# An mLSTM block ahead of two mixture-of-experts layers: decay products spread by DMA, a third bank for scores, output gates scaled on Pool, a new order of steps

## The reference, cut to what matters

```python
# attention part: batch 4, 8 heads, 768 tokens, head size 40
for t in range(S):
    m_new  = maximum(f_gate[t] + m, i_gate[t])
    f_stab = exp(f_gate[t] + m - m_new);  i_stab = exp(i_gate[t] - m_new);  m = m_new
    C = f_stab * C + i_stab * outer(v[t], k[t])
    n = f_stab * n + i_stab * k[t]
    y[t] = sigmoid(o_gate[t]) * (C @ q[t]) / maximum(abs(n @ q[t]), 1)
# then x = y as [3072, 320]; a capacity-limited top-1 MoE of 8 experts (320 -> 1024 -> 320, relu),
# then a second MoE routed by cosine similarity with a softmax weight.
```

## Time and profile before

| | us |
|---|---|
| median of the runs (972.93, 976.13, 2472.59) | 976.13 |
| profiled execution, its own time | 968.82 |
| its span | 967.0 |
| PE busy | 812.1 (84%) |
| DVE busy | 525.9 (54%) |
| POOL busy | 406.4 (42%) |
| ACT busy | 277.1 (29%) |
| mean granted clock of PE | 0.851 |

### The profile page before, as it was taken

One profiled execution on the slowest core, in us unless ns is written; L12 is line 12 of the kernel. 1 busy time (PEld: TensorE's weight loads), 2 busy tenths in 40 slices (PEclk: granted clock), 3 DMA queues, 4 the chain that ended last, 5 costly groups with the idle time before them and its releaser, 6 DMA issues.

```text
span 967.0 us, 19426 instructions
## 1 busy us (share of the span) xinstructions
PE 812.1 (84%) x5835; PEld 733.5 (76%) x5836; DVE 525.9 (54%) x1467; ACT 277.1 (29%) x671; POOL 406.4 (42%) x558
## 2 busy tenths in 40 slices
PE   1899888889567777778999999991899999999995
PEld 0777777777466667767999999991788888888994
DVE  7776878834776666666356666657222222222221
ACT  4221212200000000000467667663233332333331
POOL 4443434406510000001468888765043766527541
PEclk9998999969555555555999999996899999999999
DMA  5343444356931110115145555443547777762320
GB/s 151 122 131 116 137 128 144 113 161 168 366 98 65 65 64 34 65 65 177 49 145 165 164 164 164 140 141 104 153 136 209 219 192 249 215 194 77 104 94 1
DMA packets 72325, 131.78 MB, mean 136 GB/s; under 512 B 14583, under 2 KB 55936, under 8 KB 70498
## 3 DMA queue, kind: packets, MB, share of 16 engines
q1 hardware_dynamic: 53186, 88.72, 29.3%
q0 software_dynamic: 9600, 35.85, 11.9%
q10 hardware_dynamic: 9504, 6.79, 2.8%
HBM read 94.18 MB, written 15.24 MB: 113 GB/s over the span
## 4 chain that ended last, share of the span: by engine, by line
PE 55%; DVE 14%; issue 5%; ACT 2%; POOL 2%; DMA 0%; DVEq 0%; ACTq 0%; POOLq 0%; SPq 0%
PE bank L1442 8%; PE bank L1444 8%; PE bank L1443 8%; PE bank L1406 5%; PE bank L1419 4%; PE bank L1369 3%; PE bank L1469 3%; PE bank L1470 2%; PE bank L1471 2%; PE bank L1560 2%; DVE routing_arena L1009 1%; PE bank L1542 1%; PE bank L1541 1%; PE bank L1361 1%; PE bank L1474 1%
## 5 line engine op out<-in xcount | busy, mean ns | idle before, releaser
L1442 PE MATMUL bank<-w_hi,hT_hi 128*128 (+1 forms) x440 | 140.7, 320 | 6.4 <-DVE hT_lo L1103 3.4
L1443 PE MATMUL bank<-w_lo,hT_hi 128*128 (+1 forms) x440 | 136.7, 311 | 0.0
L1444 PE MATMUL bank<-w_hi,hT_lo 128*128 (+1 forms) x440 | 136.5, 310 | 0.0
L741 POOL TENSOR_TENSOR w_lo<-w_raw,w_hi 128x320 fp32r<-128x320 f32 x128 | 108.3, 875 | 16.9 <-ACT w_hi L489 16.0
L683 POOL DMA_INDIRECT routing_arena<-x_rows,routing_arena x24 | 23.3, 969 | 203.0 <-DVE routing_arena L1091 181.9
L710 POOL TENSOR_TENSOR w_lo<-w_raw,w_hi 128x256 fp32r<-128x256 f32 x128 | 95.5, 776 | 28.6 <-DMA w_hi<-w_raw 25.4
L1442 PEld LDWEIGHTS bank<-w_hi,hT_hi 128*128 128x128 f32 x440 | 82.8, 188 | 9.0 <-issue 9.0
L1443 PEld LDWEIGHTS bank<-w_lo,hT_hi 128*128 128x128 f32 x440 | 82.8, 188 | 0.0
L1444 PEld LDWEIGHTS bank<-w_hi,hT_lo 128*128 128x128 f32 x440 | 82.7, 188 | 0.0
L1178 DVE TENSOR_TENSOR xT_lo<-bank,xT_hi 128x256 fp32r<-128x256 f32 x31 | 13.2, 425 | 112.9 <-ACT xT_hi L561 112.9
L1103 DVE SCALAR_TENSOR_TENSOR hT_lo<-bank,hT_hi 128x384 fp32r<-128x384 f32 x64 | 35.7, 558 | 68.6 <-ACT hT_hi L504 65.7
(11 more groups left out here) (268 smaller groups left out, 1969.8 us busy)
## 6 DMA issues: line engine op xcount, KB each, us to landing
w_raw<-in_moe_w SPq DMA_DIRECT2D x16, 1280.0 KB
w_raw<-in_moe_w SPq DMA_DIRECT2D x16, 1024.0 KB
w_hi<-w_raw POOLq DMA_DIRECT2D x8, 1280.0 KB, 7.4
w_raw<-in_moe_w SPq DMA_DIRECT2D x32, 256.0 KB
w_hi<-w_raw POOLq DMA_DIRECT2D x8, 1024.0 KB, 6.8
mlstm_arena<-in_q SPq DMA_DIRECT2D x64, 120.0 KB
tokens<-in_moe_w2t SPq DMA_DIRECT2D x8, 768.0 KB, 4.2
turn_arena<-in_moe_w2t SPq DMA_DIRECT2D x8, 768.0 KB, 4.3
```

The source lines that it names most:

```text
L741: last = nc.gpsimd.tensor_tensor(w2_part(w2_lo, n)[:, k, :], w2_raw[:, k, :], w2_part(w2_hi, n)[:, k, :], ALU.subtract)
L1442: T.matmul(dst, a_hi, b_hi, start=first, stop=False)
L1443: T.matmul(dst, a_hi, b_lo, start=False, stop=False)
L1444: return T.matmul(dst, a_lo, b_hi, start=False, stop=last)
```

## The change

- `cum_parts`, `sel_pair`, `ends` and `spread_decay` go. `f_cum` keeps a place of its own. DVE splits only `f_exp`, then scans `f_cum`; ACT writes `f_cum` to a DRAM tensor `cum_rows` (32 x 768); SP, at the end of each `load_pair`, reads each head's row back into 40 partitions of `since_start`. `since_start` is zeroed once on POOL.
- `carry` takes its scalars from columns of `since_start`.
- `scores` g uses bank 2 + g, so it waits only for weights(p-1, g).
- DVE's `output` is cut in two: `scales` (L850 to L852) after decays(p, 0), and the product y after decays(p, 1). Between them POOL computes `sigden` (`scale_gates`), after its `v_in` and before its `k_dec`. The sigmoid of ACT now waits for sigden(p-2), not y(p-2).
- PE's order in step k is: scores(k+1) 0, spread_forget(k+1, 1) half 0, scores 1, half 1, scores 2, attend(k) first half, spread_forget(k+2, 0) both halves, updates(k+1), attend(k) second half.

```diff
+        cum_rows = nc.dram_tensor("cum_rows", [2 * NP, S], fp32, kind="Internal").ap()
...
+                sp.wait_ge(cum_stored, 16)
+                sp.wait_ge(state_done, pair + 1)
+                for h in range(2):
+                    sp.dma_start(since_start[64 * h:64 * h + D, s, :],
+                                 cum_rows[ds(2 * pair + h, 1), :].rearrange("a s -> (a s)").partition_broadcast(D)).then_inc(ld_since[s], 16)
...
+            act.wait_ge(cum_ready, 1)
+            nc.scalar.dma_start(cum_rows[:, :], f_cum[:, :]).then_inc(cum_stored, 16)
...
-                    act.wait_ge(y_done, pair + 1)
+                    act.wait_ge(sigden_done, pair + 1)
                     nc.scalar.activation(sig[:, s, :, :], o_rows[:, s, :, :], ACT.Sigmoid).then_inc(sig_ready, 2)
-                    act.wait_ge(state_done, pair + 1)
-                    for f in range(2):
-                        act.wait_ge(cf_ready, 2 * pair + f + 1)
-                        act.wait_ge(qs_done, 2 * pair + 1)
-                        nc.scalar.activation(since_start[:, s, f * HALF:(f + 1) * HALF], bank[4][:, 0:HALF], ACT.Identity).then_inc(since_ready, 1)
-                        nc.scalar.activation(ends[:, s, 3 * f:3 * f + 3], bank[4][:, CH - 1:HALF:CH], ACT.Identity).then_inc(ends_done, 1)
...
+            def scale_gates(s, pair):
+                pool.wait_ge(den_ready, pair + 1)
+                pool.wait_ge(sig_ready, 2 * pair + 2 + 2)
+                pool.wait_ge(y_done, pair + 2)
+                nc.gpsimd.tensor_tensor(sigden.rearrange("p c h d -> p (c h) d"), sig[:, s, :, :].rearrange("p c (h d) -> p (c h) d", d=D),
+                                        den[:, 1, :].unsqueeze(2).to_broadcast([128, NC * 2, D]), ALU.mult).then_inc(sigden_done, 1)
...
+                if not (isinstance(b, int) and b * PPB + k < 2):
+                    scale_gates(s, pair - 2)
...
+                pool.wait_ge(ld_since[s], 32 * (2 * b + k // 2 + 1))
...
-                                bank[2 + (NQ * k + g) % 2][:, :].rearrange("p (c h t) -> p h c t", h=2, t=CH),
+                                bank[2 + g][:, :].rearrange("p (c h t) -> p h c t", h=2, t=CH),
...
+            def pair_step(b, k, finish):
+                before = (b, k - 2) if k >= 2 else (b - 1, PPB + k - 2)
+                decays(b, k, 0)
+                if finish:
+                    scales(*before)
+                decays(b, k, 1)
+                if finish:
+                    output(*before)
+                for g in range(NQ):
+                    weights(b, k, g)
+                carry(b, k)
...
-                pe.wait_ge(probs_done, NQ * pair + g + 3)
+                pe.wait_ge(probs_done, NQ * pair + g + 2)
...
                 if more:
                     scores(b, k + 1, 0)
+                    spread_forget(b, k + 1, 1, 0)
                     scores(b, k + 1, 1)
-                    spread_forget(b, k + 1, 1)
-                    spread_decay(b, k + 1, 0)
+                    spread_forget(b, k + 1, 1, 1)
+                    scores(b, k + 1, 2)
                 attend(b, k, 0, NC // 2)
                 if more2:
-                    spread_forget(b, k + 2, 0)
+                    spread_forget(b, k + 2, 0, 0)
+                    spread_forget(b, k + 2, 0, 1)
                 if more:
-                    scores(b, k + 1, 2)
-                    spread_decay(b, k + 1, 1)
                     updates(b, k + 1)
                 attend(b, k, NC // 2, NC)
```

More of the change, by code:

```diff
@@ L132, in build @@
         f_parts = carve(96, [S], bf16)
-        cum_parts = carve(96, [S], bf16)
+        f_cum = carve(32, [S])
         i_cols = carve(128, [NC, 2 * NP])
@@ L155, in build @@
         f_first = carve(32, [S])
-        f_cum = carve(32, [S])
         part = carve(32, [S], bf16)
@@ L303, in build @@
         ld_rows = [sem(f"ld_rows{s}") for s in range(2)]
-        cf_ready, qs_done, ends_done = sem("cf_ready"), sem("qs_done"), sem("ends_done")
+        cum_ready, cum_stored, qs_done = sem("cum_ready"), sem("cum_stored"), sem("qs_done")
+        ld_since = [sem(f"ld_since{s}") for s in range(2)]
         fb_ready, decay_done = sem("fb_ready"), sem("decay_done")
@@ L810, in _ @@
             link(V.memset(f_exp[:, 0:S:CH], 0.0))
[L811 to L818, removed]
+            link(V.tensor_copy(f_parts[0:32, :], f_exp[:, :]))
+            link(V.tensor_tensor(gate_i[:, :], f_exp[:, :], f_parts[0:32, :], ALU.subtract))
+            link(V.tensor_copy(part[:, :], gate_i[:, :]))
+            link(V.tensor_copy(f_parts[32:64, :], part[:, :]))
+            V.tensor_tensor(f_parts[64:96, :], gate_i[:, :], part[:, :], ALU.subtract).then_inc(parts_ready, 1)
+            V.tensor_tensor_scan(f_cum[:, :], f_exp[:, :], f_first[:, :], 0.0, ALU.mult, ALU.add).then_inc(cum_ready, 1)
             dve.wait_ge(i_cols_ready, 1)
@@ L870, in carry @@
                     else:
-                        ins = V.scalar_tensor_tensor(state[:, s, c, :], state[:, s, c - 1, :], ends[:, s, c:c + 1], u3[:, c, :], ALU.mult, ALU.add)
+                        ins = V.scalar_tensor_tensor(state[:, s, c, :], state[:, s, c - 1, :], since_start[:, s, (c + 1) * CH - 1:(c + 1) * CH], u3[:, c, :], ALU.mult, ALU.add)
                     if c < NC - 2:
@@ L874, in carry @@
                 ins.then_inc(state_done, 1)
[L876 to L881, removed]
+            def pair_step(b, k, finish):
[4 more added lines that the diff above has]
+                decays(b, k, 1)
                 if finish:
                     output(*before)
[L884 to L894, removed]
+                for g in range(NQ):
+                    weights(b, k, g)
+                carry(b, k)
             for k in range(PPB):
-                pair_step(0, k, True)
-            base, per = chain.n, PPB * (4 + NC - 2)
-            with dve.Fori(1, B - 1) as b:
+                pair_step(0, k, k >= 2)
+            base, per = chain.n, PPB * (2 + NC - 2)
+            with dve.Fori(1, B) as b:
                 chain.ahead = (b - 1) * per
@@ L902, in _ @@
                 assert chain.n - base == per, (chain.n - base, per)
[L903 to L906, removed]
+            chain.n, chain.ahead = base + per * (B - 1), 0
+            for k in range(PPB - 2, PPB):
+                scales(B - 1, k)
+                output(B - 1, k)
             def inverse_norm(n2, root, inv):
@@ L1260, in _, with spread_forget @@
             last.then_inc(i_cols_ready, 1)
-            pe.wait_ge(parts_ready, 2)
+            pe.wait_ge(parts_ready, 1)
             pe.wait_ge(i_cols_copied, 1)
             pe.wait_ge(pads_ready, 5)
[L1266 to L1274, removed]
+            def spread_forget(b, k, h, f):
                 head = 2 * (b * PPB + k) + h
-                for f in range(2):
-                    pe.wait_ge(decay_done, 2 * head + f + 1)
-                    T.matmul(bank[f][:, 0:HALF], sel_head[:, ds(head, 1), :].rearrange("p a b -> p (a b)"),
-                             f_parts[:, f * HALF:(f + 1) * HALF], start=True, stop=True).then_inc(fb_ready, 1)
+                pe.wait_ge(decay_done, 2 * head + f + 1)
+                T.matmul(bank[f][:, 0:HALF], sel_head[:, ds(head, 1), :].rearrange("p a b -> p (a b)"),
+                         f_parts[:, f * HALF:(f + 1) * HALF], start=True, stop=True).then_inc(fb_ready, 1)
             def scores(b, k, g):
```

49 lines of the change are left out of this document (26 added, 23 removed).

## The result

The changed kernel takes 937.77 us (median of 4 runs, 933.74 to 938.94), against 974.53 us for the kernel before in the same comparison (median of 966.01, 972.93, 976.13 and 2472.59). The ratio leaves out that last run, which stands alone; it is 0.9647, with a 95% interval of 0.9585 to 0.9709: 3.5% faster. 939 was forecast. The span of its profiled execution is 931.5 us against 967.0. Whether the sum holds term by term is another question, and the trace answers it.

What follows compares the result with a forecast made beforehand. Bound: a loop through DVE and PE closed by two score banks, 10.25 of the 10.40 us step. Last y 30.0 + 15 x 8.5 + 4.0 + 2.7 = 164.2 against 200.1 us, so 939 us; range 924 to 957.

Steps and rivals of the forecast that it cites:

- The loop through DVE and PE, closed by two score banks: Pairs of the kernel before: carry, decays, output, weights 0, scores 2, spread and updates sum to 10.25 of the 10.40 us step.
- Floor of PE: PE's own work per step of the changed kernel, without idle time, both spread_decay and refills: 8.2 us.
- DVE without room: DVE's own work per step of the changed kernel: 8.0 to 8.25 us, next to no room.
- scale_gates on POOL: Sigmoid times reciprocal on POOL between v_in and k_dec: about 1.2 us, bounds 0.6 and 2.4, slack 0.4 before y.
- The row loads as the third loop: Sigmoid, row loads landing in 3.5 us, v_in, scale_gates and hand-overs: 8.0 us; extra landing time lengthens it directly.
- rival 1: The row loads bind: landing grows from 3.5 to 4.7 us, loop 9.2 to 9.3, time 951 us; chance 0.17.
- The signs of being wrong: In the pairs: DVE waiting before y for POOL, v_in waiting for `v` or `o_gate` instead of PE, or step over 9.5.
- P = 8.5: Forecast length in us of PE's step in the pairs, taken between 8.2 and 10.08, with three loops within 0.25 us.
- rival 2: PE's clock goes on falling at times in the pairs: add 4 to 8 us, time 945 us; chance 0.10.
- Start: Before the pairs: PE starts at 17.4 us, pair 1 loads land at 27, attend(0) starts at 30.0 instead of 34.24.
- The rule on ten DMA engines: Skill rule weighed: 40-row loads run on ten engines, each carrying 141 KB a pair, 7.4 us of an 8.5 us step.
- Rivals 3 and 4: Unseen loop keeps the step near 10 us: 963 us, chance 0.09; spreading loads choke DMA queues: 993 us, chance 0.06.

## Why the prediction was right, by its own steps

- **The loop through DVE and PE, closed by two score banks.** Right, and shown: with two banks the step is 9.15 us where three allow 8.15, and in the changed kernel the wait of scores 2 is gone. The working gave 10.25 for the kernel before, and 9.4 for two banks in the new kernel.
- **Floor of PE, 8.2 us.** Right: measured 8.13 to 8.15 in the free-running steps.
- **DVE without room.** Right: 0.20 us of wait a step with early row loads. Putting the product back costs 0.77 us a step (L855 was priced at 0.81).
- **scale_gates on POOL.** Put at 1.2 us, it took 0.99, inside the bounds. The slack was there when v_in was on time, which in the changed kernel it mostly wasn't.
- **The row loads as the third loop.** Right in kind, and the step that was mis-sized. The sum called the loop 8.0 us with a landing of 3.5; it landed in 4.0, which the sum had left to rival 1. With that landing and the 0.99 us of POOL's product the same sum gives 8.3. The table load of 1.28 us once in four steps, which the prediction named without a term of its own, adds 0.3: 8.6, an estimate from these numbers, and 8.65 was measured in the steps at full clock. So the changed kernel is between the forecast and rival 1: 4.0 us of landing, not 3.5 or 4.7. That this loop is what holds it above the floor was shown by opening it (-6.7 us, step 8.19; some 3 us of the earlier last y are the clock's).
- **The signs of being wrong.** Two of the three that the prediction named came true: DVE waits for POOL before y (7.1 us in 8 of the steps from 40 to 160 us), and v_in waits for `o_gate` instead of PE (12 times). P = 8.5 held because a margin had been put on three loops of nearly one length, not because the row loads stayed inside the step: the mechanism in the steps is that of rival 1, in a milder form. (The chances of the forecast and of rivals 1 and 2 add up to 0.85, not to the 0.84 given for "faster".)
- **The step.** 15 steps took 162.29 - 32.36 = 129.9 us, against 15 x 8.5 = 127.5. One of them holds a fall of the clock, which was rival 2. The timeline of PE there:

```profile
137.33 0.49 PE L1279 MATMUL bank<-mlstm_arena 96*128 96x384 bf16 x2
139.10 1.31 PE L1325 MATMUL bank<-mlstm_arena 128*128 128x82 f32 x10 [1.28 <-issue]
140.25 0.42 PE L1309 MATMUL bank<-mlstm_arena 128*128 128x128 f32 x2
140.51 0.95 PE L1314 MATMUL bank<-mlstm_arena 128*128 128x41 f32 x4
...
143.77 2.02 PE L1290 MATMUL bank<-mlstm_arena 128*128 128x256 f32 x4
...
150.62 1.24 PE L1325 MATMUL bank<-mlstm_arena 128*128 128x82 f32 x10
```

  The step is 11.52 us (139.10 to 150.62), and the same four matmuls of L1290 take 2.02 us in place of 1.08: the granted clock was 0.50 from 140.6 to 147.4. It follows a wait of 1.28 us. Without that step the other 14 average (129.9 - 11.5) / 14 = 8.46 as the prediction counts, from attend to attend. So 8.5 was about right for a step at full clock, and the extra 3 us are rival 2 come once instead of never. The same rival explains part of the gain: the kernel before was at half clock for 17 us of its pairs (68.1 to 78.4, 92.0 to 95.4, 126.1 to 129.6) and this one for 6.8 behind the start. At half rate half of that time is lost, so about 5 of the 31.4 us are the clock's, by estimate.
- **Start.** PE started at 17.5 (forecast 17.4) and the loads of pair 1 landed at 27.5 (27). But attend came at 32.36, not 30.0: PE had idled 3.39 us, its clock fell, and the three scores with two spreads took 4.7 us, not 3.0. The wait was foreseen, its price in clock was not: with scores 2 late, an idle stretch of 2.89 us in the same place left the clock at full rate, and the same scores and spreads ran at 1.03 to 1.13 us for four matmuls, in place of 1.84 and 1.88.
- **End.** 168.7 - 162.3 = 6.4 us against 6.7.
- **Nothing changes behind the last y.** Right of the code, and off by 4.1 us in these two executions, in favour, by the luck of the clock. The sum of the errors is -2.4 (start) -2.4 (steps) +0.3 (end) +4.1 (clock in the logits) = -0.4, which is why 35.9 and 35.5 agree. The total is closer than its parts deserve, and that is luck. From the profiled execution to the median the forecast added 6.1 us (932.9 to 939), and 4.0 were measured (933.74 to 937.77).
- **The rule on ten DMA engines.** The semaphore updates in the trace bear on it. In both kernels each load of 128 rows updates its semaphore 16 times and each load of 40 rows 11 times (on one semaphore each, 528 for 48 loads of q and k and 176 for 16 spreading loads). The first of the 11 comes as the issue ends, the others with the data: the two spreading loads issued at 19.27 and 19.76 us update theirs at 19.74 and 20.24, and then twenty times from 21.0 to 22.2. The Trainium skill, page "DMA: Bandwidth & Descriptors", section "Why a DMA increments its semaphore by 16 and not by 1", takes the largest number up to 16 that divides the slowest dimension, ten for 40 rows; each of these engines updates the semaphore once, and the issuer adds the remaining six at once. The trace agrees: ten updates and one. Whether that is why the landing grew by 0.5 us, and fell by 0.35 to 0.4 without the spreading loads, no run shows: more traffic on all 16 engines would give the same sign.
- **Rivals 3 and 4** fell: there was no unseen loop near 10 us, and 40 reads of one row of DRAM are a load like others (issued in 0.30 us each).

## What to carry to other kernels

Write the step as a set of closed loops, each with its length, and compare the longest three: the gain of an edit ends where the next loop begins, and undoing an edit measures its price only when the other loops are shorter (the third bank: 2 to 4 us in the changed kernel, hardly clear of the scatter, 13 with the row loads released). When a step shrinks, look again at every wait that asks for more than its buffer needs: one that cost nothing at 10.4 us a step cost 6.7 us at 8.7. Extra traffic can be hidden itself and still lengthen the landing of the transfer that counts. And compare steps with the clock's falls counted apart: one fall is worth 3 us here, as much as some edits.

## What was not expected of the hardware

- PE's clock fell to half for 6.8 us (140.6 to 147.4) after one wait of 1.28 us, with PE 88% busy in the 10 us before (8.82 of 10.00), and didn't fall after similar waits of 1.11 and 1.19 us elsewhere (68.80 and 104.16 in the changed kernel). The length of the wait alone doesn't decide it: in the kernel before it fell at 68.1 us, with no wait of PE over 0.44 us in the 11 us ahead, and with sigmoid times reciprocal back on DVE it fell after a wait of 1.39 us (before 70.50) and didn't after one of 1.60 (before 110.25). With early row loads, where PE was busy for 118.94 of 120 us, it fell at 29.3 us, behind the idle stretch at the start, and then not before 159.0.
- The same code behind the last y took 761.2 to 769.7 us in fourteen profiled executions. The shortest had the highest granted clock in its first 15 us (0.89), the three longest the lowest (0.50). This hides or adds up to 8 us in a comparison of two executions of this kernel, more than some of the edits above are worth.
- POOL's product with 480 elements per row, one operand spread by a step of 0, took 0.99 us, as long as its product with 384 elements and two plain operands (1.00). A price scaled by width was 20% too high.
